# Attention scores from 64-row products on plain and swapped copies

## The reference, cut to what matters

```python
q_rot, k_rot = rotate(q), rotate(k)            # (4, 8, 576, 64) each
scores = (q_rot @ k_rot.transpose(0, 1, 3, 2)) / sqrt(64)
attn = exp(scores - scores.max(-1)); attn = attn / (attn.sum(-1) + 1e-9)
x = (attn @ v).transpose(0, 2, 1, 3).reshape(4 * 576, 512)
h = x @ w_in                                   # (2304, 2048)
g = maximum(h, 0) + alpha * minimum(h, 0)
return g @ w_out                               # (2304, 512)
```

## Time and profile before

| | |
|---|---|
| median of 3 runs | 691.19 us |
| profiled execution, its own time | 693.63 us |
| its span, first to last instruction | 691.8 us |
| granted TensorE clock, mean | 0.994 of full speed |
| TensorE busy | 678.7 us (98%) |
| VectorE, ScalarE, GpSimd busy | 337.6, 339.6, 268.6 us |
| chain that ended last | TensorE 95% of the span |
| of it, score products (L567) | 12% |
| DMA copies of high and low parts, median time to landing | 2.4 us (queries), 2.9 us (keys) |

### The profile page before, as it was taken

One profiled execution on the slowest core, in us unless ns is written; L12 is line 12 of the kernel. 1 busy time (PEld: TensorE's weight loads), 2 busy tenths in 40 slices (PEclk: granted clock), 3 DMA queues, 4 the chain that ended last, 5 costly groups with the idle time before them and its releaser, 6 DMA issues.

```text
span 691.8 us, 13444 instructions
## 1 busy us (share of the span) xinstructions
PE 678.7 (98%) x4664; PEld 575.1 (83%) x4664; DVE 337.6 (49%) x779; ACT 339.6 (49%) x794; POOL 268.6 (39%) x258
## 2 busy tenths in 40 slices
PE   7799999999999999999999999999999999999998
PEld 7677777777777776698889999999999999999996
DVE  5677776777766676345642343233234322333222
ACT  2788888888888887333332222322322232223223
POOL 5655777777775505022222222222222222222222
PEclk9999999999999999899999999999999999999999
DMA  6898666666666645300001000000000000001001
GB/s 155 201 244 205 152 147 139 157 146 146 149 145 135 138 107 181 137 0 2 1 1 45 1 1 17 31 1 1 30 15 0 0 30 15 0 0 46 1 1 45
DMA packets 76882, 51.35 MB, mean 74 GB/s; under 512 B 61348, under 2 KB 61732, under 8 KB 76324
## 3 DMA queue, kind: packets, MB, share of 16 engines
q1 hardware_dynamic: 76402, 50.26, 29.0%
q10 hardware_dynamic: 434, 0.49, 0.3%
HBM read 22.95 MB, written 4.72 MB: 40 GB/s over the span
## 4 chain that ended last, share of the span: by engine, by line
PE 95%; SPq 1%; DVE 1%; ACT 1%; DMA 1%; issue 0%; POOL 0%
PE banks L698 29%; PE banks L727 29%; PE banks L567 12%; PE banks L646 10%; PE banks L603 6%; PE banks L621 6%; PE banks L642 3%; DMA k_two<-k_hi 1%; ACT prob L769 0%; DMA cos_sb<-in_cos 0%; ACT pt L816 0%; DVE prob L951 0%; SPq L347 0%; SPq L327 0%; SPq L345 0%
## 5 line engine op out<-in xcount | busy, mean ns | idle before, releaser
L504 POOL TENSOR_TENSOR g_lo<-g,g_hi 128x384 fp32r<-128x384 f32 (+1 forms) x98 | 99.7, 1018 | 312.9 <-ACT g_hi L889 303.5
L1064 DVE TENSOR_SCALAR g<-banks,alpha_sb 128x384 f32<-128x384 f32 (+1 forms) x98 | 59.7, 610 | 251.0 <-ACT pos L880 251.0
L880 ACT ACTIVATE pos<-banks 128x384 f32<-128x384 f32 x96 | 47.1, 491 | 170.2 <-PE banks L698 170.2
L698 PE MATMUL banks<-x_hi,w_in_hi 128*128 128x384 f32 x384 | 129.5, 337 | 0.0
L698 PE MATMUL banks<-x_hi,w_in_lo 128*128 128x384 f32 x384 | 129.3, 337 | 0.0
L698 PE MATMUL banks<-x_lo,w_in_hi 128*128 128x384 f32 x384 | 129.1, 336 | 0.0
L727 PE MATMUL banks<-w_out_hi,g_hi 128*128 128x512 f32 x288 | 114.8, 399 | 0.3
L727 PE MATMUL banks<-w_out_hi,g_lo 128*128 128x512 f32 x288 | 112.9, 392 | 0.0
L727 PE MATMUL banks<-w_out_lo,g_hi 128*128 128x512 f32 x288 | 111.9, 388 | 0.0
L889 ACT ACTIVATE g_hi<-g 128x384 fp32r<-128x384 f32 (+1 forms) x98 | 50.9, 519 | 115.9 <-DVE g L1067 115.9
L951 DVE TENSOR_SCALAR_CACHE_REDUCE prob<-banks 128x576 f32<-128x576 f32 x128 | 93.1, 754 | 25.9 <-PE banks L567 24.1
(11 more groups left out here) (92 smaller groups left out, 902.9 us busy)
## 6 DMA issues: line engine op xcount, KB each, us to landing
k_two<-k_hi SPq DMA_DIRECT2D x62, 160.0 KB, 2.9
out<-stage SPq DMA_DIRECT2D x18, 256.0 KB, 2.0
raw_q<-in_q SPq DMA_DIRECT2D x32, 128.0 KB, 2.7
raw_k<-in_k SPq DMA_DIRECT2D x32, 128.0 KB, 2.5
q_two<-q_hi SPq DMA_DIRECT2D x32, 128.0 KB, 2.4
q_two<-q_lo SPq DMA_DIRECT2D x32, 128.0 KB, 2.4
q_own<-q_hi SPq DMA_DIRECT2D x32, 128.0 KB, 2.4
raw_v<-in_v SPq DMA_DIRECT2D x32, 128.0 KB, 2.3
```

The lines of the kernel that those rows point to most:

```text
L504: nc.gpsimd.tensor_tensor(g_lo[f % 2][:, part], g[f % 2][:, part], g_hi[f % 2][:, part].bitcast(F32), ALU.subtract).then_inc(g_lo_done, 1)
L698: mm = nc.tensor.matmul(h_ps[f % 2], w[:, j, cols], xx[:, j, :], start=(step == 0), stop=(step == 3 * CT - 1))
L880: nc.scalar.activation(pos[f % 2][:, :], h_ps[f % 2], ACT.Relu).then_inc(pos_done, 1)
L1064: nc.vector.tensor_scalar(g[f % 2][:, part], h_ps[f % 2][:, part], 0.0, alpha_sb[:, f:f + 1], ALU.min, ALU.mult).then_inc(neg_done, 1)
```

## The change

The stacked copies go. Queries and keys of a pair are kept as `q_nat` and `k_nat` (high and low part side by side in one buffer, two pairs in turn; the remainder queries are columns of `q_nat`), and a copy with the two halves of the partitions exchanged, `q_swap` and `k_swap`, is made by four transfers in place of ten (`swap` for `stack`). An A or B tile is made of 3 x 2 products of 64 rows; the first half of the keys is taken on partitions 0 to 63, the second on 64 to 127, by turns, each in its own bank as before. For head 0 the lower rows come from the plain and the upper from the swapped copies, for head 1 the other way round. The remainder tile and the first tiles of period 0 keep their products.

The orders change too. U_MIXED goes behind U_K (numbers, transposes, splits), with other banks for both. In a period's lists, VectorE takes U_PB[3] and U_PA[2] for U_PB[1], ScalarE U_PB[1] for U_PB[3] and U_PA[2]; the copy of U_PA[3] goes behind the last exponential; the splits of the queries and the maxima are ordered anew. In the opening, both key copies are SP's.

```diff
-U_Q, U_MIXED, U_K = 7, 8, 9
+U_Q, U_K, U_MIXED = 7, 8, 9
...
-            def stack(p, par, side):
+            def swap(p, par, side):
                 if side == 0:
-                    two, on_own, on_other, arrived = q_two[par], q_hi, q_lo, q_two_in
                     sp.wait_ge(evac[U_Q % T_BANKS], evac_count(p - 1, U_Q))
+                    dst, cols, arrived = q_swap[par], (slice(0, QT * P), slice(0, QT * P)), q_swap_in
+                    src = q_nat[par]
                 else:
-                    two, on_own, on_other, arrived = k_two[par], k_hi[par], k_hi[par], k_two_in
                     sp.wait_ge(evac[U_K % T_BANKS], evac_count(p - 1, U_K))
                     sp.wait_ge(evac[U_MIXED % T_BANKS], evac_count(p - 1, U_MIXED))
-                for head, (own, other) in enumerate(((slice(0, D), slice(D, P)), (slice(D, P), slice(0, D)))):
-                    sp.dma_start(two[own, head, :].bitcast(F32), on_own[own, :].bitcast(F32)).then_inc(arrived, 16)
-                    sp.dma_start(two[other, head, :].bitcast(F32), on_other[own, :].bitcast(F32)).then_inc(arrived, 16)
-                    if side == 0:
-                        sp.dma_start(q_own[par][own, head, :].bitcast(F32),
-                                     q_hi[own, :].bitcast(F32)).then_inc(arrived, 16)
+                    dst, cols, arrived = k_swap[par], (slice(0, HALF), slice(REM + HALF, REM + S)), k_swap_in
+                    src = k_nat[par]
+                for to, of, keys in ((LOW, HIGH, cols[0]), (HIGH, LOW, cols[1])):
+                    sp.dma_start(dst[to, :, :].bitcast(F32), src[of, :, keys].bitcast(F32)).then_inc(arrived, 16)
...
+        SPLIT = ((HI, HI), (HI, LO), (LO, HI))
...
-                    products = ((q_two[par][block], k_two[par][:, head, :]), (q_own[par][block], k_lo[par]))
-                for j, (lhs, rhs) in enumerate(products):
-                    for h in range(2):
-                        mm = nc.tensor.matmul(tile[:, h, :], lhs[:, :], rhs[:, first + h * HALF:first + (h + 1) * HALF],
-                                              start=(j == 0), stop=(j == len(products) - 1))
+                head, i = divmod(n - 1, QT)
+                of_q = slice(i * P, (i + 1) * P)
+                if head == 0:
+                    sides = ((LOW, q_nat[par], k_nat[par], slice(REM, REM + HALF)),
+                             (HIGH, q_swap[par], k_swap[par], slice(0, HALF)))
                 else:
+                    sides = ((LOW, q_swap[par], k_swap[par], slice(0, HALF)),
+                             (HIGH, q_nat[par], k_nat[par], slice(HALF, S)))
+                for j, (qx, kx) in enumerate(SPLIT):
+                    for h, (rows, q_of, k_of, keys) in enumerate(sides):
+                        mm = nc.tensor.matmul(tile[:, h, :], q_of[rows, qx, of_q], k_of[rows, kx, keys],
+                                              start=(j == 0), stop=(j == len(SPLIT) - 1))
...
                 turn(p, t, U_Q)
                 score(p, t, A_TILES[2])
-                turn(p, t, U_MIXED)
                 score(p, t, A_TILES[3])
                 if not is_opening(p):
                     turn(p, t, U_K)
+                    turn(p, t, U_MIXED)
...
                 flat(p, U_PB[0], t)
+                flat(p, U_PB[1], t)
                 exps(p, t, REM_TILE)
                 flat(p, U_PB[2], t)
-                flat(p, U_PB[3], t)
...
                 exps(p, t, B_TILES[1])
-                flat(p, U_PA[2], t)
-                flat(p, U_PA[3], t)
                 exps(p, t, B_TILES[2])
                 exps(p, t, B_TILES[3])
+                flat(p, U_PA[3], t)
...
                 maxima(p, t, A_TILES[0])
                 maxima(p, t, A_TILES[1])
-                if has_now(p):
-                    reciprocals(p, t, 2)
+                flat(p, U_PB[3], t)
+                lo(p, U_Q, t)
                 maxima(p, t, A_TILES[2])
-                lo(p, U_Q, t)
                 maxima(p, t, A_TILES[3])
-                lo(p, U_MIXED, t)
                 if not is_opening(p):
                     lo(p, U_K, t)
+                    lo(p, U_MIXED, t)
...
                 maxima(p, t, B_TILES[2])
+                flat(p, U_PA[2], t)
                 maxima(p, t, B_TILES[3])
```

More of the change, by code:

```diff
@@ L209, in build @@
         x_hi[1] = sb(ctx, "x_hi1", [P, CT, CHUNK], F32R)
-        sb(ctx, "gap", [P, (until_prob - used[0]) // 4])
+        if until_prob > used[0]:
+            sb(ctx, "gap", [P, (until_prob - used[0]) // 4])
         g = [sb(ctx, f"g{i}", [P, CHUNK]) for i in range(2)]
@@ L315, in build, with q_rem @@
         IN_LOAD = (16 * 4, 16 * 2)
+        def q_rem(par, r, part):
+            return q_nat[par][r, part, QT * P + r.start:QT * P + r.stop]
         @block.sync
@@ L370, in _ @@
             load(1, 1)
[L371 to L375, removed]
+            swap(0, 0, 0)
+            swap(0, 0, 1)
             def batch(b):
@@ L461, in _ @@
                 nc.gpsimd.memset(raw[0:REM, QT, D:P], 0.0).then_inc(padded, 1)
[L462 to L467, removed]
+            for nat in q_nat:
+                nc.gpsimd.memset(nat[LOW, :, QT * P + REM:QT * P + P].bitcast(F32), 0.0).then_inc(padded, 1)
+                nc.gpsimd.memset(nat[HIGH, :, QT * P:QT * P + REM].bitcast(F32), 0.0).then_inc(padded, 1)
             pool.wait_ge(padded, PADDED)
@@ L549, in score @@
                 tile, par = s_ps[(t * TILES + n) % 2], t % 2
[L550 to L556, removed]
-                else:
[L558 to L562, removed]
-                    products = ((q_two[par][block], k_two[par][:, head, :]), (q_own[par][block], k_lo[par]))
@@ L565, in score @@
-                for j, (lhs, rhs) in enumerate(products):
-                    for h in range(2):
-                        mm = nc.tensor.matmul(tile[:, h, :], lhs[:, :], rhs[:, first + h * HALF:first + (h + 1) * HALF],
-                                              start=(j == 0), stop=(j == len(products) - 1))
+                ahead = isinstance(p, int) and p == 0
+                if n == REM_TILE or (ahead and n in FIRST_TILES):
+                    if n == REM_TILE:
+                        of_q, rows = slice(QT * P, QT * P + P), slice(0, P)
+                    else:
+                        of_q, rows = slice((n - 1) * P, n * P), LOW
+                    for j, (qx, kx) in enumerate(SPLIT):
+                        for h in range(2):
+                            mm = nc.tensor.matmul(tile[:, h, :], q_nat[par][rows, qx, of_q],
+                                                  k_nat[par][rows, kx, REM + h * HALF:REM + (h + 1) * HALF],
+                                                  start=(j == 0), stop=(j == len(SPLIT) - 1))
+                    mm.then_inc(scored, 1)
+                    return
@@ L777, in hi @@
                 bank = t_ps[u % T_BANKS]
+                nx = (t + 1) % 2
                 if u == U_Q:
-                    if not (isinstance(p, int) and p < 0):
-                        act.wait_ge(q_two_in, (p + 1) * Q_STACKED)
-                    if isinstance(p, int) and p == 0:
-                        act.wait_ge(scored, FIRST_TILES[-1] + 1)
-                    jobs = [(q_hi[:, :], bank, SCALE)]
+                    jobs = [(q_nat[nx][:, HI, 0:QT * P], bank, SCALE)]
                 elif u == U_K:
-                    jobs = [(k_hi[(t + 1) % 2][:, REM:S], bank, 1.0)]
+                    jobs = [(k_nat[nx][:, HI, REM:S], bank, 1.0)]
                 else:
-                    jobs = [(qrem_hi[r, r], bank[r, 0:REM], SCALE) for r in HEADS]
-                    jobs.append((both_ends(k_hi[(t + 1) % 2]), bank[:, REM:P].unsqueeze(1)
+                    jobs = [(q_rem(nx, r, HI), bank[r, 0:REM], SCALE) for r in HEADS]
+                    jobs.append((both_ends(k_nat[nx][:, HI, :]), bank[:, REM:P].unsqueeze(1)
                                  .to_broadcast([P, 2, REM]), 1.0))
@@ L838, in period @@
                 hi(p, U_Q, t)
-                hi(p, U_MIXED, t)
-                twice(p)
-                if not is_opening(p):
-                    exps(p, t, A_TILES[0])
-                exps(p, t, A_TILES[1])
+                exps(p, t, A_TILES[0])
                 if not is_opening(p):
                     hi(p, U_K, t)
+                    hi(p, U_MIXED, t)
+                twice(p)
+                exps(p, t, A_TILES[1])
                 exps(p, t, A_TILES[2])
@@ L908, in _ @@
                 hi(-1, u, -1)
-            act.wait_ge(evac[U_K % T_BANKS], evac_count(-1, U_K))
-            act.wait_ge(evac[U_MIXED % T_BANKS], evac_count(-1, U_MIXED))
-            for own, head, other in ((slice(0, D), 0, slice(D, P)), (slice(D, P), 1, slice(0, D))):
-                act.dma_start(k_two[0][other, head, :].bitcast(F32), k_hi[0][own, :].bitcast(F32)).then_inc(k_two_in, 16)
             def batch(b):
```

64 lines of the change are left out of this document (33 added, 31 removed).

## The result

The changed kernel takes **680.46 us** (median of 4 runs, 679.42 to 682.43); the kernel before took 691.26 beside it. The ratio is 0.9837, with a 95% interval of 0.9801 to 0.9874: 10.8 us faster. Forecast were 672.5 and 18.65 less. The sign was right; the time is inside the wide range (667 to 686) and outside the likeliest case's own (668 to 677.5).

The account below looks back on a forecast made before the run. TensorE's list was taken to bound each period: 16.35 - 1.06 - 0.15 + 0.10 = 15.24, over 15 periods 16.65, with 1.6 (opening) and 0.4 (end) 18.65 saved, giving 672.5 us; own range 668 to 677.5, wide range 667 to 686.

Parts of the forecast that it names:

- likeliest case: Whole kernel: the forecast of 672.5 us, own range 668 to 677.5, chance 0.63.
- Part 1: Score tiles: products on the two row halves overlap completely, 0.1325 a pair, 0.40 a tile; 1.06 us saved a period.
- R2: Score pairs: the load path serves one half at a time, 0.22 a pair; 704.5 us, or 720 without product overlap; chance 0.09.
- R4: Score pairs: the halves overlap only in part, 0.15 to 0.177 a pair; 680 to 690 us; chance 0.08.
- R3: Score pairs: a half's load waits until that half's product is through, 0.245 a pair, 0.73 a tile; 712 us; chance 0.03.
- Part 2: TensorE's changes between 64 and 128 rows: four old ones go (0.45), three new come (0.30); net 0.15 saved a period.
- Part 3: Hand-offs from ScalarE and VectorE to the faster TensorE: three places get thin; 0.10 a period charged, bounds 0 and 0.7.
- R1: Periods: late hand-offs at three thin places stall TensorE, 0.6 a period; 680 us, up to 685; chance 0.17.
- Part 4: Transfers: ten become four, SP's queue free some 3.6 us sooner a period; a steady period gains nothing, no cover lost.
- Part 5: Opening: KREM transposes of the second period at 28.6 for 30.25; 1.6 us saved, bounds 0.3 and 2.2.
- Part 6: Period without scores: one of two successive ScalarE copies goes to VectorE; 0.4 us saved, bounds 0 and 1.

Follow-up runs that it names:

- e3: Changed kernel, but a score tile's three products on the lower 64 rows are queued first, then the three on the upper; 680.0 us, ratio 0.9814.
- e8: Changed kernel with all four A tiles made of six products on the lower 64 rows alone, from the plain copies; 702.91 us, ratio 1.0131.
- e9: New products and transfers under the engine orders of the kernel before, plus products of zeros to hold the clock up; 685.07 us, ratio 0.9897.
- e1: New products and transfers with all engine orders as in the kernel before, no added products of zeros; 692.82 us, ratio 0.9985.
- e6: The kernel of e5b with the INV transposes also moved ahead of the fifth tile; 680.38 us, ratio 0.9799.
- e5b: Repeat of the filled kernel: changed kernel plus products of zeros where TensorE waits in the opening and last period; 677.94 us, ratio 0.9793.
- e0: The changed kernel run again with no edit, for its spread; 681.1 us, ratio 0.9817.
- e2: Kernel before, with its old products and ten transfers, given the new engine orders; 692.66 us, ratio 0.999.
- e4: Changed kernel with the INV transposes moved from behind the sixth tile to ahead of the fifth; 683.4 us, ratio 0.9842.
- e11: On e10: in the opening, VectorE takes the eighth tile's maximum before the copy of U_PA[2] instead of after; 676.98 us, ratio 0.9758.
- e10: On the kernel of e5b: in the opening, keys and MIXED are turned and split between the fifth and sixth tiles; 677.64 us, ratio 0.9789.

## Why the prediction was right in sign and too large

**Part 1, right.** Pairs every 0.13, in one order of products and in the other (e3), and e8 loses some 21 us where half the tiles give it up. R2 and R4 are out: neither the two loads nor the products of a pair hold each other. R3 is out too; the rule of the Trainium skill behind it (TensorE: Matmul & The Clock Gate, Part 3, The mechanism) would have made a tile 0.73, and the trace shows two in 0.93.

**Part 2, the step that failed in the period.** I took 0.45 for the four old changes of mode and 0.30 for three new ones, 0.15 saved. Stretch by stretch against the old period, with 0.13 a tile taken off for part 1: the U_PB transposes with their two tiles give 0.19 and the U_PA ones 0.14, together 0.33 of the 0.45. From the queries' transposes to the products with the values it takes 2.35 (127.85 to 130.20 above) where the kernel before took 2.19:

```profile
131.58 0.66 PE L603 MATMUL banks<-ident,rot_q 128*128 128x128 f32 x4
131.99 0.50 PE L567 MATMUL banks<-k_two,q_two 128*128 128x288 f32 x2
...
133.77 0.65 PE L642 MATMUL banks<-pt,raw_v 128*128 128x288 f32 x2
```

Two tiles lie there, so 0.26 should have gone: the place costs 0.42 more (0.36 in periods where GpSimd splits no weights, 2.29), and I had priced its two changes at 0.20 together. Before, a tile followed these transposes 0.41 after their start; now 0.59. The sixth tile's change cost 0.15, for the 0.10 I gave it. Net 0.24 lost for 0.15 saved, 0.39 a period. The bound was 0.15 lost, and mis-summed: with none of the four old prices gone, the three new ones would have made it 0.30. How much of the 0.42 is the change of mode and how much the moved MIXED was not tried separately. e9 has a price for a change: MIXED between two tiles, two changes more, costs 0.27 to 0.34 (2.62 to 2.64 for 2.29 to 2.36), some 0.13 to 0.17 each.

**Part 3, the hand-offs.** The charge of 0.10 was not used up: from 52 to 240 no product of TensorE waits for ScalarE or VectorE, and four weight loads wait 0.7 in all. R1's mechanism is real all the same: with the old orders it comes at the second A tile (e1, e9), and e6 brings it out with one unit moved. The new orders keep it away, but that is the smaller part of their 7.1 us (half of the 14.4 that the filled kernel gains, 692.29 to 677.94). Against e5b, e9 loses some 0.37 at the second A tile in six periods, 2.2 us; at MIXED's place between the tiles it loses 4.3 us in fourteen periods, and that is part 2's term. So a period is 15.24 + 0.39 - 0.10 = 15.53 by these terms, and 15.55 in the trace where GpSimd also splits the dense layer's weights (15.44 where it doesn't: 208.47 to 223.91). Fifteen periods: 12.49 for 16.65, 4.16 missing.

**Part 4** held as far as seen: the DMA share fell, and TensorE waits for no transfer in the periods, before or after.

**Part 5, wrong in sign:** 1.6 forecast, 1.35 lost, 2.95 missing. The copies came in time as said (19.01; I had 18.5). Three steps failed. First, K comes 0.9 later than walked (21.63 for 20.7) and the splits end at 24.33 instead of 23.1: TensorE stands 2.04 and the U_PA transposes start at 24.44, 1.24 later than forecast. Second, from there to KREM I had 5.4. With the clock at 1.00 it takes 6.08 (e3, 24.33 to 30.41; 6.07 in e5b), 0.68 more, and took 5.98 before. I counted ScalarE's list as one copy shorter and didn't look where VectorE's extra copy stands: ahead of the last maximum. Third, the clock was not in the working: behind the gap it fell to its lower level, 1.2 GHz, until about 33, and the same stretch took 7.16, 1.08 more. The three make the 3.0 by which KREM misses 28.6. The third doesn't come each time: behind a gap of 2.04 the clock fell in the profiled executions of the kernel after, e0, e2 and e8 and stayed up in those of e3 and e4; behind 1.46 it stayed up in that of before and fell in that of e1. ScalarE and VectorE of the kernel after:

```profile
29.90 0.78 ACT L777 ACTIVATE prob<-prob,nmax 128x576 f32<-128x576 f32 x1 [1.36 <-DVE prob L948]
```

```profile
28.50 0.69 DVE L995 COPY pt<-banks 128x512 f32<-128x512 f32 x1 [1.52 <-PE banks L628]
29.11 0.75 DVE L948 TENSOR_SCALAR_CACHE_REDUCE prob<-banks 128x576 f32<-128x576 f32 x1
```

e11 exchanges the two and KREM comes at 29.73; with both mended the opening gains 0.5 on the kernel before, not 1.6. Some 0.46 of the rest is held back by the products of zeros (e10, by estimate); why what remains stays out was not tried.

**Part 6, mis-sized:** 3.06 for 0.4, mostly by the clock, of which nothing was forecast. TensorE's waits ahead of those products hardly shrank (1.94 in four before, 1.91 in three after). The kernel before had fallen to half clock from about 278 to 285 in its profiled execution, and the kernel after did not in this one. With the clock at 1.00 in both, the old orders take 414.71 from KREM of the last period to the end (e9), the new ones 414.44 (e5b): some 0.3 of the 0.4.

Together 18.65 - 4.16 - 2.95 + 2.66 = 14.2, the profiled difference; that part 6's surplus makes up for most of part 5 is luck of the two executions. The medians differ by only 10.8 because the runs of both kernels vary with how long the half clock lasts. Of the kernel before, beside e5b, five runs at a mean clock of 1.00 took 690.7 to 691.76, four at 0.998 took 692.81 to 693.4, one at 0.995 took 696.57; the nine runs of the changed kernel (with e0) all lie at 0.990 to 0.997. With the clock at 1.00 on both sides (691.59, the middle one of those five, and e5b's 677.94, with its products of zeros) the difference is 13.7 of the 18.65 forecast. No run of the kernel before was filled. That the time came out inside the wide range is owed to part 1 and to the width of the range; parts 2 and 5 came out against it.

## What to carry to other kernels

Two products on different halves of the rows ran at the price of one here (a pair in 0.13), so halving the rows of each pays where six short ones replace four long ones. But count every place where the list goes between 64 and 128 rows at both ends, and look for what stands there: one unit between two such tiles cost 0.27 to 0.34 a period, 4.3 us in all. When TensorE gets faster, go through the other engines' lists anew, and ask of each moved copy which reduction it now stands in front of (0.6 us in one opening, e11). And a gap of 2 us on TensorE costs more than itself when the clock falls behind it: a few products of zeros, there and in the last period, were worth 2.4 us here. Fit their number to the gap: once it had shrunk, they held TensorE up (e10).

## What the runs showed of the hardware

- Products queued three and three on the two halves start in twos, so a later one of the free half begins before earlier ones of the busy half (e3). The Trainium skill (TensorE: Matmul & The Clock Gate, Part 3, The mechanism) has products as strictly first in, first out; the starts in this trace, and the unchanged time of 680.0, say otherwise for different row groups.
- TensorE can stand for 5.1 us (2.22 + 2.92) between two periods, waiting for nothing that the profile shows, with three packets on the instruction queue, while ScalarE and VectorE wait for it (e1). With twelve products added elsewhere it didn't come (e9: 685.07 for 692.82, the products' own gain included). What decides it stays open.
- The same gap of TensorE, 2.04 us, was followed by half clock in four profiled executions and by full clock in two (part 5).
